# Turning the expert inputs on VectorE instead of TensorE, in a fused attention and mixture-of-experts kernel

## What is computed

```python
h = np.maximum(x[b, s] @ w1[e], 0.0)      # 512 -> 1024
out[b, s] = p[e] * (h @ w2[e])            # 1024 -> 512
```

## Time and profile before

| what | value |
|---|---|
| median of three runs | 418.8 us |
| the profiled execution, its time | 419.02 us |
| its span (first to last instruction) | 416.9 us |
| TensorE busy | 405.5 us, 97% of the span |
| VectorE, ScalarE, GpSimd busy | 55%, 50%, 25% |
| mean granted TensorE clock | 0.997 |
| DMA, mean over the span | 162 GB/s |

### The profile page before, as it was taken

One profiled execution on the slowest core, in us unless ns is written; L12 is line 12 of the kernel. 1 busy time (PEld: TensorE's weight loads), 2 busy tenths in 40 slices (PEclk: granted clock), 3 DMA queues, 4 the chain that ended last, 5 costly groups with the idle time before them and its releaser, 6 DMA issues.

```text
span 416.9 us, 7057 instructions
## 1 busy us (share of the span) xinstructions
PE 405.5 (97%) x2597; PEld 342.1 (82%) x2598; DVE 228.8 (55%) x293; ACT 209.7 (50%) x293; POOL 105.1 (25%) x104
## 2 busy tenths in 40 slices
PE   7999999999999999999999999999999999999992
PEld 3888799887889987879788888888888888888881
DVE  4788739973004879477376511106961273655640
ACT  2334678670214865380557423327852563747640
POOL 3344873000000000026622212213232222322320
PEclk9999999999999999999999999999999999999998
DMA  8999900000520007753474711015691173572500
GB/s 291 406 412 415 396 6 2 0 2 0 201 91 12 2 0 314 292 192 109 169 290 150 328 50 50 26 50 201 269 416 54 44 307 155 181 291 64 222 17 25
DMA packets 16152, 67.74 MB, mean 162 GB/s; under 512 B 2623, under 2 KB 4159, under 8 KB 11776
## 3 DMA queue, kind: packets, MB, share of 16 engines
q1 hardware_dynamic: 12928, 58.87, 35.9%
q0 software_dynamic: 2912, 8.13, 5.7%
q10 hardware_dynamic: 288, 0.41, 0.3%
...
## 4 chain that ended last, share of the span: by engine, by line
PE 92%; DMA 5%; SPq 1%; ACT 1%; issue 0%; POOL 0%; DVE 0%; POOLq 0%; ACTq 0%
PE ps L996 26%; PE ps L998 25%; PE ps L997 25%; DMA kv<-qkv 5%; PE ps L1262 4%; PE ps L1236 2%; PE ps L1047 2%; PE ps L1044 2%; PE ps L1026 1%; PE ps L1093 1%; PE ps L1010 1%; PE ps L1072 0%; PE ps L1168 0%; PE ps L1102 0%; PE ps L1159 0%
## 5 line engine op out<-in xcount | busy, mean ns | idle before, releaser
L929 DVE TENSOR_TENSOR hT<-ps,hT 128x512 fp32r<-128x512 f32 x34 | 23.5, 691 | 88.5 <-ACT hT L643 88.5
L916 DVE TENSOR_TENSOR wx<-raw_w,wx 128x1024 fp32r<-128x1024 f32 x56 | 65.1, 1218 | 2.8 <-ACT wx L584 1.6
L996 PE MATMUL ps<-wx,hT 128*128 128x512 f32 x136 | 56.1, 413 | 0.3 <-issue 0.3
L584 ACT CAST wx<-raw_w 128x1024 fp32r<-128x1024 f32 x56 | 55.0, 1049 | 0.0
L996 PE MATMUL ps<-wx,xT 128*128 128x512 f32 x136 | 54.7, 402 | 0.2 <-DVE xT L952 0.2
L998 PE MATMUL ps<-wx,xT 128*128 128x512 f32 x136 | 53.2, 391 | 0.0
L998 PE MATMUL ps<-wx,hT 128*128 128x512 f32 x136 | 53.1, 391 | 0.0
L997 PE MATMUL ps<-wx,xT 128*128 128x512 f32 x136 | 53.0, 390 | 0.0
L997 PE MATMUL ps<-wx,hT 128*128 128x512 f32 x136 | 53.0, 390 | 0.0
L996 PE MATMUL ps<-x,win 128*128 128x384 f32 x128 | 43.2, 337 | 0.0
L998 PE MATMUL ps<-x,win 128*128 128x384 f32 x128 | 42.8, 334 | 0.0
(11 more groups left out here) (162 smaller groups left out, 760.0 us busy)
## 6 DMA issues: line engine op xcount, KB each, us to landing
raw_w<-w_exp SPq DMA_DIRECT2D x28, 1024.0 KB, 4.7
qk<-qkv SPq DMA_DIRECT2D x7, 768.0 KB, 9.7
raw_first<-w_exp SPq DMA_DIRECT2D x4, 1024.0 KB, 8.0
kv<-qkv SPq DMA_DIRECT2D x4, 768.0 KB, 11.5
x_rows<-x2n SPq DMA_DIRECT2D x11, 256.0 KB, 2.8
...
x_early<-x2n SPq DMA_DIRECT2D x10, 256.0 KB, 2.3
...
```

Of the source, the lines that this page charges most:

```text
L584: nc.scalar.copy(wx[:, slot, 0, c], raw).then_inc(wx_hi[w], 1)
L916: nc.vector.tensor_tensor(wx[:, slot, 1, c], raw, wx[:, slot, 0, c].bitcast(F32), ALU.subtract).then_inc(w2_lo_dve if w else w1_lo_dve, 1)
L929: nc.vector.tensor_tensor(lo, psHT[:, 512 * a:512 * a + 512], hi.bitcast(F32), ALU.subtract).then_inc(hT_done, 1)
L996: mm(o, lh, rl, start=first, stop=False)
```

## The change

- `gather(g)` still fills `xg`, but one block further ahead. SyncE's new `step(g)` stores `xg` (block g+2) to a DRAM buffer `x_block`, waits until it has landed, and reloads it by four DMAs into `xq`: quarter q of the columns goes to partitions 32q to 32q+31, where j of 32 partitions takes the tokens j, 32+j, 64+j and 96+j.
- VectorE's `turn_x` turns the 32x32 squares of `xq` into `xF` (features on partitions, in SBUF). `x_hi` and `x_lo` read `xF` and come after `h_hi(g, 1)` and `h_lo(g, 1)`. In TensorE's step `turn_x` is gone.
- The features lie in another order so; W1 is laid out for it on the host (`quarters`).
- `turn_h(g, 0)` moves two matmuls earlier and `turn_h(g, 1)` one later, into the middle of a group of three.
- `first_rows`, `last_rows` and the turn for block 1 (`turn_second`, from its own buffer `x1g`) become plain matmuls on 32 columns at a time, four for each one before. `x2_half` takes 64 of every 128 columns instead of 256 in one piece, and so does the store of the last rows.
- In `first_w1` the order of parts changes; of block 0's W2, piece 2 of lo goes from GpSimd to VectorE.
- In the first block of an expert ScalarE's `evac_before` moves behind `relu(g, 0)`, and W1's piece 3 behind `h_hi(g, 0)`.
- GpSimd gathers before it scatters. SyncE's loads follow the experts' block loops now: W2 of e+1 ahead of expert e's first step, W1 of e+3 after its last.

```diff
+TR = 32
+NQ = P // TR
...
     x2_early = nc.dram_tensor("x2_early", (T - 2 * P, DM), F32, kind="Internal").ap()
+    x_block = nc.dram_tensor("x_block", (P, DM), F32, kind="Internal").ap()
     KB = 1024
...
     hs = at("hs", [P, FF], F32, 140)
+    xF = at("xF", [P, KD, P], F32, 192)
+    xq = at("xq", [P, NQ, P], F32, 196)
     os_ = at("os", [P, DM], F32, 194)
+    x1g = at("x1g", [P, DM], F32, 192)
...
+
+        def column_half(a, n):
+
+            return a.rearrange("t (q n c) -> t n q c", q=NQ, n=2)[:, n]
...
             for n in range(2):
-                h = slice(DM // 2 * n, DM // 2 * n + DM // 2)
                 sp.wait_ge(x2_out, TT + n)
-                sp.dma_start(x2_rows[T - P:T, h], x2n[:, (TT - 1) % 3, h]).then_inc(x2_stored[(TT - 1) % 3], 16)
+                sp.dma_start(column_half(x2_rows[T - P:T, :], n), column_half(x2n[:, (TT - 1) % 3, :], n)
+                             ).then_inc(x2_stored[(TT - 1) % 3], 16)
                 if n == 0:
...
                     raw(1, 1, raw_w2, raw_w2_in, (0,))
+            def step(g):
+
+                sp.wait_ge(gathered, 16 * g + 48)
+                sp.wait_ge(x_turned, 16 * g + 48)
+                sp.dma_start(x_block, xg[:]).then_inc(x_stored, 16)
+                sp.wait_ge(x_stored, 16 * g + 16)
+                for q in range(NQ):
+                    sp.dma_start(xq[TR * q:TR * q + TR],
+                                 x_block[:, P * q:P * q + P].rearrange("(b j) n -> j b n", j=TR)
+                                 ).then_inc(quartered, 16)
+
+            def raw_w2_next(e):
+
+                sp.wait_ge(w2_lo_dve, 4 * e)
+                raw(1, e, raw_w2, raw_w2_in)
+
+            def raw_w1_next(e, s):
+
+                sp.wait_ge(w1_lo_dve, 4 * e + 7)
+                raw(0, e + 3, raw_w1[s], raw_w1_in[s])
+
...
             raw(1, 1, raw_w2, raw_w2_in, (1,))
+            sp.wait_ge(x_first, 2)
+            step(0)
             raw(0, 2, raw_w1[0], raw_w1_in[0])
-            sp.wait_ge(w2_lo_pool, 3)
-
-            def raw_w2_next(e):
-
-                sp.wait_ge(w2_lo_dve, 4 * e)
-                raw(1, e, raw_w2, raw_w2_in)
-
-            def raw_w1_next(e, s):
-
-                sp.wait_ge(w1_lo_dve, 4 * e - 5)
-                raw(0, e, raw_w1[s], raw_w1_in[s])
-
-            with sp.Fori(2, E - 2, 2) as ee:
-                raw_w2_next(ee)
-                raw_w1_next(ee + 1, 1)
-                raw_w2_next(ee + 1)
-                raw_w1_next(ee + 2, 0)
-            raw_w2_next(E - 2)
-            raw_w1_next(E - 1, 1)
-            raw_w2_next(E - 1)
+            sp.wait_ge(w2_lo_pool, 2)
+
+            def expert(e, s, ahead):
+
+                first, end = block_range(sp, e)
+                if not (isinstance(e, int) and e == 0):
+                    if ahead > 0:
+                        raw_w2_next(e + 1)
+                    step(first)
+                rest(sp, first, end, step)
+                if ahead > 2:
+                    raw_w1_next(e, 1 - s)
+
+            sp.wait_ge(tables, 1)
+            expert(0, 0, 3)
+            with sp.Fori(1, E - 4, 2) as ee:
+                expert(ee, 1, 3)
+                expert(ee + 1, 0, 3)
+            expert(E - 3, 1, 2)
+            expert(E - 2, 0, 1)
+            expert(E - 1, 1, 0)
...
         def _(pool):
-            pool.sem_inc(xg_free, 1)
-
...
-                pool.wait_ge(xg_free, g + 1)
...
             def step(g):
+                pool.wait_ge(x_stored, 16 * g)
+                gather(g + 2)
                 scatter_before(g)
-                pool.wait_ge(gathered, 16 * g + 32)
-                gather(g + 2)
...
             pool.wait_ge(gathered, 16)
-            pool.wait_ge(xg_free, 2)
             nc.gpsimd.tensor_copy(gnow[:], gidx[:, 1:2]).then_inc(g_copied, 1)
...
             nc.gpsimd.indirect_dma_start(
-                xg[:], None, x2_rows, bass.IndirectOffsetOnAxis(gnow[:, 0:1], 0)).then_inc(gathered, 16)
-            weights_lo(1, 0, 0, (1, 2))
+                x1g[:], None, x2_rows, bass.IndirectOffsetOnAxis(gnow[:, 0:1], 0)).then_inc(gathered, 16)
+            weights_lo(1, 0, 0, (1,))
+            pool.wait_ge(gathered, 32)
+            pool.wait_ge(xg_read, 1)
+            gather(2)
             pool.wait_ge(tables, 1)
-            pool.wait_ge(gathered, 32)
-            gather(2)
...
                 bounds_check=T - 1, oob_is_err=False).then_inc(scattered, 16)
+            pool.wait_ge(quartered, 64 * end)
             pool.wait_ge(gathered, 16 * end + 32)
...
-            def x_hi(g):
-
-                act.wait_ge(xg_free, g + 2)
-                nc.scalar.copy(xT[:, 0].rearrange("p k t -> p (k t)"), psXT).then_inc(xT_hi, 1)
+            def x_hi(g, source):
+
+                nc.scalar.copy(xT[:, 0].rearrange("p k t -> p (k t)"), source).then_inc(xT_hi, 1)
...
                 relu(g, 1)
-                x_hi(g + 1)
                 h_hi(g, 1)
+                act.wait_ge(x_turned, 16 * g + 48)
+                x_hi(g + 1, xF[:].rearrange("p k t -> p (k t)"))
...
+                relu(g, 0)
                 evac_before(g, o_done)
-                relu(g, 0)
+                h_hi(g, 0)
                 if e is not None:
                     weights_hi(0, e, slot, (3,))
-                h_hi(g, 0)
                 relu(g, 1)
-                x_hi(g + 1)
                 h_hi(g, 1)
+                act.wait_ge(x_turned, 16 * g + 48)
+                x_hi(g + 1, xF[:].rearrange("p k t -> p (k t)"))
...
                 act.wait_ge(x2_done, TT + n)
-                h = slice(DM // 2 * n, DM // 2 * n + DM // 2)
-                nc.scalar.copy(x2n[:, (TT - 1) % 3, h], psXh[n]).then_inc(x2_out, 1)
+                nc.scalar.copy(column_half(x2n[:, (TT - 1) % 3, :], n),
+                               psXh[n].rearrange("t (q c) -> t q c", q=NQ)).then_inc(x2_out, 1)
                 act.wait_ge(x_first, n + 1)
...
             relu(0, 1)
-            x_hi(1)
+            act.wait_ge(x1_turned, 1)
+            x_hi(1, psXT)
             h_hi(0, 1)
...
         def _(dve):
-            dve.sem_inc(w2_lo_dve, 3)
+            dve.sem_inc(w2_lo_dve, 2)
+            dve.sem_inc(x_turned, 48)
             nc.vector.memset(warm[:], 0.0).then_inc(made, 1)
...
-            def x_lo(g):
+            def turn_x(g, waited):
+
+                dve.wait_ge(quartered, waited)
+                nc.vector.transpose(xF[:].rearrange("p k (q t) -> p k q t", q=NQ),
+                                    xq[:].rearrange("p q (k i) -> p k q i", k=KD)).then_inc(x_turned, 16)
+
+            def x_lo(g, source):
                 dve.wait_ge(xT_hi, g + 1)
-                nc.vector.tensor_tensor(xT[:, 1].rearrange("p k t -> p (k t)"), psXT,
+                nc.vector.tensor_tensor(xT[:, 1].rearrange("p k t -> p (k t)"), source,
                                         xT[:, 0].rearrange("p k t -> p (k t)").bitcast(F32),
...
             def step(g):
                 h_lo(g, 0)
-                x_lo(g + 1)
+                turn_x(g + 1, 64 * g)
                 h_lo(g, 1)
+                x_lo(g + 1, xF[:].rearrange("p k t -> p (k t)"))
...
                 h_lo(g, 0)
+                turn_x(g + 1, 64 * g)
                 if e is not None:
                     weights_lo(0, e, slot, (3,))
-                x_lo(g + 1)
                 h_lo(g, 1)
+                x_lo(g + 1, xF[:].rearrange("p k t -> p (k t)"))
...
                                         ALU.subtract).then_inc(x0_lo if n == 0 else xT_done, 1)
+            weights_lo(1, 0, 0, (2,))
             h_lo(0, 0)
-            x_lo(1)
+            x_lo(1, psXT)
             h_lo(0, 1)
...
-            def three(o, lh, ll, rh, rl, first, last):
+            def three(o, lh, ll, rh, rl, first, last, amid=None):
...
+                if amid:
+                    amid()
...
             def x2_half(n, k):
                 ts = slice(S - P, S)
-                ws = slice(DM * k + DM // 2 * n, DM * k + DM // 2 * n + DM // 2)
-                last = three(psXh[n], hg[:, 0, k, ts], hg[:, 1, k, ts], wout[:, 0, ws], wout[:, 1, ws],
+                wh, wl = (column_half(wout[:, w, DM * k:DM * k + DM], n) for w in range(2))
+                last = three(psXh[n].rearrange("t (q c) -> t q c", q=NQ), hg[:, 0, k, ts], hg[:, 1, k, ts], wh, wl,
                              k == 0, k == KF - 1)
...
                 for k in parts:
-                    ins = mm(psX0[:, k, :], x2n[:, t % 3, P * k:P * k + P], oh0[:, t - TT + 2, :], start=False,
-                             stop=True, skip_group_check=True)
+                    for q in range(NQ):
+                        ins = mm(psX0[TR * q:TR * q + TR, k, :], x2n[:, t % 3, P * q + TR * k:P * q + TR * k + TR],
+                                 oh0[:, t - TT + 2, :], start=False, stop=True, skip_group_check=True)
                     if t == TT - 1 and k % 2 == 1:
...
                 for k in range(KD):
-                    last = nc.tensor.transpose(psX0[:, k, :], xg[:, P * k:P * k + P], ident)
```

(54 more changed lines are left out.)

12 lines of the change are left out of this document (7 added, 5 removed).

## The result

The changed kernel takes 421.76 us (median of 9 runs, 419.93 to 423.83) beside 418.98 us for the kernel before (9 runs, 418.48 to 419.65): a ratio of 1.0068, 95% interval 1.0048 to 1.0089. It is slower by 2.8 us; 413.8 was forecast, in a range from 412.2 to 416.4. The profiled execution took 423.83 us with a span of 421.6 us at a mean granted clock of 0.989 (before: 419.02, 416.9, 0.997). So it is the upper end of the runs: it shows 4.8 us of loss where the medians show 2.8.

The account below looks back on a forecast made before the run. TensorE, busy 97% of the span, was taken to bound the kernel; -7.0 (turns) + 2.0 - 0.3 (seam) + 0.35 (pause) = -5.0 us gives 414.0, or 413.8 against the median; range 412.2 to 416.4.

Parts of the forecast that it names:

- The relay by DRAM: SyncE's store and quarters each block: quarters in 6.2 us after the turn, slack 5.6; gather slack 4.5; cost nothing.
- What queues behind SyncE's new waits is only the raw W2 and W1: SyncE's queue: W1 of e+3 issued after a step, an expert's length ahead of use; W2 keeps its wait; cost nothing.
- a crowd of transfers after block 7: Rival: W2 and W1 of two experts plus relay delay store and quarters, costing up to 2 us, say 415.8; chance 0.17.
- The relay is slower than a block: Rival: quarters landing late set the block's length instead of TensorE; at Q = 7.5, 9 us on top, 422.8; chance 0.06.
- 16 turns of x: Expert stage: transposes of x leave TensorE's steps, 16 x 0.44 us = 7.0 us gained; a block becomes 11.83 us.
- The seam: Up to block 1: transposes become small matmuls at 37 ns, +2.0 us, less 0.31 of removed waiting: +1.7 us.
- The last rows in runs of 256 B: Store before the second gather: 1.1 us longer costs 0.2, as long as before nothing; taken as nothing.
- The doubling: Store before the second gather: if read-modify-write doubled 1.7 us, the gather is 1.7 late and the sum 0.8 us higher.
- VectorE's transpose: turn_x on VectorE in each step: 0.6 us, in the idle time between the two h_lo; cost nothing.
- The pause at block 8: After block 7, where VectorE is full: its h_lo comes late and TensorE stands 0.35 us, once.
- The slacks within a step: Each block: 0.28 us left between relu of half 1 and its turn, 0.47 for half 1 of turned h.

Follow-up runs that it names:

- e4: Changed kernel with raw weight loads cut to an eighth from W1 of expert 3 and W2 of expert 2 on, so wrong weights; 413.92 us.
- e8: e5 with one edit: W1 for expert 4 issued one block later, behind the step of expert 1's second block; 414.65 us.
- e11: Changed kernel with one fetch moved: W1 of expert 3 behind block 2's step instead of block 1's; 415.71 us.
- e1: Changed kernel with raw W1 fetched two experts ahead, behind raw W2 and before the expert's first step; 426.99 us.
- e5: Changed kernel with W1 of e+3 behind expert e's first step if more blocks follow, otherwise behind the next expert's first step; 419.88 us.

## Why the prediction was wrong

**The step that failed** is the last of the sum, "The relay by DRAM", costed at "Nothing". It has three faults, and all are of one kind: each transfer was given the time it has in quiet.

- The gather was taken at 2.5 us behind 1.0 of issue, and the chain of store, gather and its slack of 4.5 from that. Beside the 2 MB of W1 for expert 2 it took 8.14 us, issue and all, instead of 3.5, and `step` 1 began its store at 226.11; SyncE had the quarters out at 229.9 and reached W1 for expert 3 at 230.13. That alone costs nothing: in e4, e8 and e11 the same store begins at 225.0 to 225.7, hardly earlier.
- "What queues behind SyncE's new waits is only the raw W2 and W1" was right in its list and wrong in its price. W1 for expert 3 and W2 for expert 2 stand next to each other in SyncE's program, and the step's waits held W1 back until both went out in one burst: ScalarE waited 7.85 us for W2. The kernel before had W2 ahead of W1.
- ScalarE's program was not followed behind that wait. `relu` of an expert's second block stands behind W2's pieces, so a late W2 reaches TensorE within a few microseconds (3.92), and the pause brings the lower clock behind it (2.66 more).

The rival "a crowd of transfers after block 7" had the crowd, with a chance of 0.17, but let it hurt by another path, a late store and late quarters, and looked only at blocks 7 to 9 and at 2 us. There these blocks cost 3.4 us (1.47 + 1.92) in this execution, 0.8 of it the pause that e4 has too, and TensorE waited there for `relu`, behind W2 in ScalarE's program; the path by the quarters is the one of e1 and e5. The larger loss, 6.7 us, is at blocks 2 to 4, where the relay starts up, and the prediction didn't look there: it worked out the relay in its steady state alone. "The relay is slower than a block" gave nearly the right time, 422.8, for a reason that didn't occur: the quarters are late in 3 blocks of 16, by 3.1 us in all.

**The other terms held.** In the order of the prediction:

- 16 turns of x of 0.44 us leave TensorE, and an undisturbed block is 11.81 to 11.88 us, forecast 11.83.
- The seam. Its small matmuls after:

```profile
196.38 1.01 PE ps L1228 x32
197.39 0.87 PE ps L1217 x32
...
198.81 0.57 PE ps L1217 x16
```

  27 to 36 ns each, where 37 was taken from the earlier trace rows: 1.01 and 0.87 instead of 1.18 and 1.18, 0.57 instead of 0.59. The first turn of h in block 1 starts 1.24 us later than before (216.93 to 218.17). Of that, 0.25 were there before the seam (196.13 to 196.38), and this turn now stands two matmuls, 0.46, earlier in its block: 1.24 - 0.25 + 0.46, some 1.5 us net for the seam, forecast 1.7.
- The last rows in runs of 256 B are stored in 2.2 to 2.5 us instead of 1.7, and the weight load of the second turn waits 0.4 us for the gather behind them. The doubling that the prediction worked out beside the Trainium skill's rule (DMA: Bandwidth & Descriptors, Specifications) didn't come; that such runs are slower did.
- VectorE's transpose takes 0.70 us, forecast 0.6, and hides as it should:

```profile
262.26 0.70 DVE L959 STREAM_TRANSPOSE xF<-xq 128x512 f32<-128x512 f32 x1
```

- The pause at block 8 was to be 0.35. Where nothing else disturbs (e4), blocks 7 to 8 and 8 to 9 are 0.30 and 0.50 over 11.83, 0.8 together: the one compute term that was too small, by 0.45. VectorE's `h_lo` accounts for 0.17 of it there; the chain also runs through ScalarE's pieces and its `relu`, which the prediction had not followed. The seam, 0.25 too dear, makes up for half of that by luck.
- The slacks within a step (0.28 and 0.47) held in every undisturbed block.

**The account.** In the profiled execution the first turn of h in the last block starts at 405.8 instead of 401.1, 4.7 us later. That is 0.8 before block 0, 0.46 more until block 1 (12.64 in place of 12.18; block 1's turn of x is still TensorE's), minus 15 x 0.44 = 6.6, plus the 10.1 of the four disturbed blocks: 4.8. And e4, with these gone, is 4.9 us faster than before, where the sum said 5.0. The prediction's sum is a forecast of e4, not of the change.
